# Two half-height products side by side: the low remainder of two width tiles on the two halves of TensorE's rows

## What is computed

```python
def _moe2_ref(x, domain_probs, w1, w2):          # x: 3072 x 320, E = 4, F = 1024
    p = domain_probs / (domain_probs.sum(-1, keepdims=True) + 1e-09)
    for e in range(E):
        h = np.maximum(x @ w1[e], 0.0)
        out += p[:, e:e + 1] * (h @ w2[e])
    return out
```

## Time and profile before

| | us |
|---|---|
| median of 3 runs (lowest, highest) | 1663.45 (1659.49, 1669.53) |
| profiled execution, its own time | 1664.84 |
| span of the profiled execution | 1663.1 |
| first matmul of the experts to the end of the span | 966.86 to 1663.1 |
| one steady step of the experts | 14.35 |

### The profile page before, as it was taken

The page is one execution under the profiler, slowest core; times in us unless marked ns, Lnnn a source line. Parts: engine busy times, 40 slices in busy tenths (PEclk is TensorE's granted clock), DMA queues, the critical chain, the costliest instruction groups (busy, mean ns, idle before and its releaser), DMA issues. The chain is left out here.

```text
span 1663.1 us, 37883 instructions
## 1 busy us (share of the span) xinstructions
PE 1484.1 (89%) x15888; PEld 1295.1 (78%) x15888; DVE 811.2 (49%) x1396; ACT 420.4 (25%) x859; POOL 374.4 (23%) x314
## 2 busy tenths in 40 slices
PE   2387688998989999999969779999999999999998
PEld 1266566877877877877868679999999999999998
DVE  7959765776865955853211323333333333333333
ACT  1123343343333233333223311111111111111111
POOL 4122553332332322321233340202020202020000
PEclk9978798999998988998989889999999999999999
DMA  6545684065066135111010420101010100000011
GB/s 183 163 129 144 161 216 109 17 179 145 11 161 159 31 109 133 37 56 41 9 35 1 147 70 0 35 0 35 0 35 0 34 0 18 17 0 0 0 47 47
DMA packets 89411, 112.84 MB, mean 68 GB/s; under 512 B 10952, under 2 KB 67400, under 8 KB 89288
## 3 DMA queue, kind: packets, MB, share of 16 engines
q1 hardware_dynamic: 89288, 111.05, 24.2%
HBM read 78.73 MB, written 32.28 MB: 67 GB/s over the span
## 5 line engine op out<-in xcount | busy, mean ns | idle before, releaser
L1443 PE MATMUL banks<-x2t,u 128*128 x1536 | 377.6, 393 | 8.4 <-POOL u L1410 8.4
L1453 PE MATMUL banks<-u,hid 128*128 128x320 f32 x2304 | 360.6, 309 | 0.0
L1453 PEld LDWEIGHTS banks<-u,hid 128*128 128x128 f32 x2304 | 349.0, 188 | 11.2
L1508 DVE SCALAR_TENSOR_TENSOR hid<-banks,hid 128x512 fp32r<-128x512 f32 x192 | 132.7, 691 | 414.0 <-ACT hid L1478 414.0
L1443 PEld LDWEIGHTS banks<-x2t,u 128*128 128x128 f32 x1536 | 284.2, 189 | 61.3 <-issue 8.6
L1478 ACT ACTIVATE hid<-banks 128x512 fp32r<-128x512 f32 x192 | 115.0, 599 | 581.5 <-PE banks L1443 581.5
L859 PE MATMUL banks<-xt,wi 128*128 128x512 f32 x768 | 197.6, 400 | 20.5 <-issue 12.8
L868 PE MATMUL banks<-wo,hid 128*128 128x320 f32 x1152 | 183.8, 309 | 5.6 <-POOL hid L1283 5.6
L868 PEld LDWEIGHTS banks<-wo,hid 128*128 128x128 f32 x1152 | 175.4, 188 | 14.1 <-POOL hid L1283 6.4
L859 PEld LDWEIGHTS banks<-xt,wi 128*128 128x128 f32 x768 | 142.3, 191 | 48.4 <-issue 13.9
L1283 POOL TENSOR_TENSOR hid<-shared,hid 128x512 fp32r<-128x512 f32 x96 | 123.5, 1287 | 226.8 <-ACT hid L1011 226.5
(11 more groups left out here) (112 smaller groups left out, 1553.3 us busy)
## 6 DMA issues: line engine op xcount, KB each, us to landing
scaled_operands<-made SPq DMA_DIRECT2D x41, 416.8 KB
made<-kbaw SPq DMA_DIRECT2D x41, 312.0 KB
kb<-scaled_operands SPq DMA_DIRECT2D x24, 416.0 KB
raw<-w SPq DMA_DIRECT2D x8, 640.0 KB, 5.6
lam<-scaled_operands SPq DMA_DIRECT2D x24, 209.6 KB
at<-scaled_operands SPq DMA_DIRECT2D x24, 208.0 KB
raw<-w SPq DMA_DIRECT2D x8, 512.0 KB, 4.0
rt<-rvt SPq DMA_DIRECT2D x96, 40.0 KB
```

The source lines that it names most:

```text
L1443: mm = pe.matmul(p_up[f][:], u1[:, par, w, f * 128:(f + 1) * 128], xt[:, x, cols], start=(i == 0), stop=(i == 7))
L1453: mm = pe.matmul(p_dn[t][:, 0:D], hid[:, f, h, t * 128:(t + 1) * 128], u2[:, par, w, f, :], start=(f == 0 and i == 0), stop=(f == NFU - 1 ...
L1508: dve.scalar_tensor_tensor(out=hid[:, f, 1, :], in0=p_up[f][:], scalar=0.0, in1=hid[:, f, 0, :].bitcast(F32), op0=ALU.max, op1=ALU.subtract)\
```

## The change

The pass (LO2, ST2) of every `up` is taken out, and `up` has seven passes. In its place `remainders(f)` is called once for each pair of tiles, after up 0 and after up 2: one matmul on rows 0 to 63 for tile f (low weights x `ST2`, whose upper half is the tokens' high part) and one on rows 64 to 127 for tile f + 1 (low weights x a new slot `BELOW`, whose lower half is a copy of the high part), into the two banks `p_up[f]` and `p_up[f + 1]`. The product of the low weights and the tokens' low part, which the pass before had along with it, is left out. The first of the two ends the group of tile f and signals `e_up`; the second opens the group of tile f + 1, which its `up` ends. ScalarE makes one copy more per chunk in the turning stage. TensorE's steps are written out for the six chunks and the two halves, and only the loop over the 4 experts is left.

```diff
-        xt = sb("x2t", [128, 5, NT * 128], F32R)
+        xt = sb("x2t", [128, 6, NT * 128], F32R)
...
+                    if k == 2 and c >= 2:
+                        pe.wait_ge(below_saved, c - 1)
...
-            passes = [(HI0, HI0), (HI0, LO0), (LO0, HI0), (HI1, HI1), (HI1, LO1), (LO1, HI1), (ST2, ST2), (LO2, ST2)]
+            pe.wait_ge(below_saved, NCH)
+
+            passes = [(HI0, HI0), (HI0, LO0), (LO0, HI0), (HI1, HI1), (HI1, LO1), (LO1, HI1), (ST2, ST2)]
...
-                cols = bass.ds(n * TOK, TOK)
+                cols = slice(n * TOK, (n + 1) * TOK)
...
-                                       start=(i == 0), stop=(i == 7))
-                    mm.then_inc(e_up, 1)
+                                       start=(f % 2 == 0 and i == 0), stop=(f % 2 == 1 and i == 6))
+                    if f % 2:
+                        mm.then_inc(e_up, 1)
+
+                def remainders(f):
+
+                    for s, x in ((0, ST2), (1, BELOW)):
+                        half = slice(64 * s, 64 * s + 64)
+                        mm = pe.matmul(p_up[f + s][:], u1[half, par, LO2, (f + s) * 128:(f + s + 1) * 128],
+                                       xt[half, x, cols], start=(s == 1), stop=(s == 0))
+                        if s == 0:
+                            mm.then_inc(e_up, 1)
...
                 up(0)
+                remainders(0)
                 for f in range(1, NFU):
                     up(f)
+                    if f % 2 == 0:
+                        remainders(f)
                     down(f - 1)
                 down(NFU - 1)
 
-            blocks(pe.Fori, step)
+            with pe.Fori(0, NE) as e:
+                for par in range(2):
+                    for n in range(NCH):
+                        step(e, par, n, (2 * e + par) * NCH + n)
...
+                    if k == 2:
+                        act.activation(xt[64:128, BELOW, c * TOK:(c + 1) * TOK], TURN[c % 2][k][64:128, :], ACT.Copy)\
+                            .then_inc(below_saved, 1)
```

More of the change, by code:

```diff
@@ L48 @@
 HI0, HI1, LO0, LO1, ST2, LO2 = range(6)
+BELOW = LO2
 INV_STEPS = 3 + 2 * (BLK - 1) + 1
@@ L1341, in experts @@
         cleared = sem("sum_cleared")
+        below_saved = sem("x2_remainder_below_saved")
         block = ctx.enter_context(nc.Block())
```

## The result

The changed kernel takes 1688.7 us (median of 6 runs, 1680.04 to 1692.93), the kernel before 1661.89 in the same six rounds. The ratio is 1.0156, 95% interval 1.0123 to 1.0189: slower by 1.6%, or 26.8 us. The forecast was 28.6 us on the median (1663.45 to 1692), with a range of 1669 to 1713.

A forecast was written before the change was run, and what follows sets the result against it. The prediction took TensorE to bound the experts. To the profiled 1664.84 us it added 25.9 for the pairs and 3 for the jumps, giving 1693.7, or 1692 against the median of 1663.45; range 1669 to 1713.

The forecast's parts named there:

- TensorE is the bound, and the pitch is the price: Experts: the stage ends when TensorE ends; every 0.1 us lost per pair of tiles costs 9.6 us.
- The saving, one matmul per pair: Each pair of tiles: two half-height matmuls run side by side, saving one matmul, 0.23 us.
- Way in, way out, bare load behind: Around each pair: 0.09 us in, 0.09 out, 0.11 for up 1's bare load and 0.01 for the next interval.
- The pair's own loads: Pair's two fp32r weight loads, not made ahead: 0.20 us, bounds 0 and 0.22, scaled from fp32 rows.
- The jumps: Three jumps back over twelve written-out TensorE steps: 1 us each, 3 in all, ends 0 and 6.6.
- the cover: At each far jump: TensorE's program can be past the last down early, hiding at most 2.0 us.
- the fetch: At each far jump: code fetched when asked for, up to a small transfer's landing, 2.2 us.
- The turning stage is covered: Turning stage: six more ScalarE copies add at most 3.6 us, to 963.5; PE waits until 966.86, so no cost.
- The two loads are not bare: Rival: the pair's loads are made during the way in; +0.07 us per pair, 6.7 us, 1672 with jumps; chance 0.15.
- The changes of tiling are hidden: Rival: only the pairs' saving is left, 21 us saved, 1645 after the jumps; chance 0.07.
- Not side by side in fp32r: Rival: the half-height pair doesn't overlap in fp32r; another 0.22 us per pair, 21 us, 1713; chance 0.12.
- The jumps cost more: Rival: the jumps or a late down 0 cost 10 us or more on top, 1702 and above; chance 0.07.

The follow-up runs named there:

- both on the same rows: Changed kernel with the expert loop also written out (no jumps), both half-height matmuls of a pair on rows 0 to 63: 1699.3 us against 1658.76 before.
- four at once: Changed kernel without jumps, all four half-height matmuls of a step together at its head: 1665.63 us against 1662.39 for the kernel before.
- the two kernels that have them: The changed kernel, 1688.7 us, and the kernel before with only its TensorE steps written out, expert loop kept, 1667.76 us against 1658.76.

## Why the prediction was right, and where it was off

- **TensorE is the bound, and the pitch is the price.** Right: PE had no wait in the experts but at the start and at the jumps, and the step lengths add up to the difference.
- **The saving, one matmul per pair.** Right. Both start within 0.01 us, and on the same rows it is 0.23 us more.
- **Way in, way out, bare load behind.** Right: 0.32 and 0.34 as in the earlier trace rows, where they had been read off a place with plain fp32 on the half rows. The way out, 0.43 less the load's 0.11 and the pitch of 0.23, is 0.09 as forecast, and it stands alone in two experiments (both on the same rows, four at once) with 0.32 against 0.23.
- **The pair's own loads**, the term that no row showed, was put at 0.20 and is 0.11. The step that failed is "0.11 x 0.10 / 0.06": the 0.10 us of L721 were read as two loads one behind the other, and measured against the 0.06 us of L1427 as one. With a single half-height matmul the interval is the same 0.43, so two loads on different rows are not bare for longer than one. The trace of before had it too, in the rows of the loads:

```profile
799.57 0.19 PEld L721 LDWEIGHTS banks<-rt,shared 40*128 40x128 f32 x2 [0.36 <-issue]
...
799.68 0.19 PEld L721 LDWEIGHTS banks<-rt,shared 40*128 40x128 f32 x2
...
948.25 0.14 PEld L1427 LDWEIGHTS banks<-ident,x 128*128 128x128 f32 x1
```

The first two loads of L721 start together at 799.57, and the next two 0.11 us later: its 0.10 us are one load's time, not two. What differs is L1427, a transpose, whose second load starts 0.06 us behind its first at 948.19; why that is half as long no run shows. The net loss per pair is 0.19 us instead of 0.27, 18.2 us instead of 25.9.
- **The jumps** were put at 1 us each, 3 in all, with 6.6 as the upper end, and cost 8.0 to 9.5. Both the cover and the fetch were off. The block that is fetched starts only 0.75 to 0.85 us before `up` is due, where the forecast had a cover of up to 2.0 us, and from its start to the first matmul it takes 2.6 to 3.0 us, where a small transfer had 2.2. The difference is the 1.8 to 2.2 us of wait. And a second part was not in the forecast at all: the clock. Behind three of the six jumps in the two kernels that have them TensorE ran at 0.50 for some 3 to 4 us, which cost another 1.6 or 1.7 us each. The two errors are of opposite sign (7.7 us too much, 6.5 too little). That the sum is so close, 28.6 forecast and 26.8 measured, is luck.
- **The turning stage is covered.** Right, and with 4.0 us to spare where 3.4 were forecast:

```profile
949.95 0.69 DVE L1524 TENSOR_TENSOR x2t<-banks,x2t 64x512 fp32r<-64x512 f32 x1 [0.20 <-ACT x2t L1496]
...
951.77 2.89 POOL L1412 TENSOR_TENSOR u<-raw,u 128x1280 fp32r<-128x1280 f32 x1
...
954.80 3.35 PE L1448 MATMUL banks<-x2t,u 128*128 128x512 f32 x7 [6.82 <-POOL u L1412]
```

VectorE's last subtraction ends at 950.64, POOL's split at 954.66, and PE starts at 954.80.

- **The rivals.** "The two loads are not bare" (+0.07 per pair) fell: +0.19, one load bare. (By its own terms it stood at 1663.45 + 6.7 + 3 = 1673, not 1672.) "The changes of tiling are hidden" fell: they are paid in full although the neighbours are matmuls of 512 columns. "Not side by side in fp32r" fell by the run with both on the same rows. "The jumps cost more" came true in part, with 6.5 us on top instead of 10 or more.

The Trainium skill, "TensorE: Matmul & The Clock Gate", Part 3, gives a pack the time of one matmul and some 4 ns for each further tile. The pair itself agrees (starts within 0.01 us); what it costs where it stands alone, 0.43 us to the next matmul, is more. The Trainium skill, "Runtime: NRT & Kernel Launch", Instruction fetch mechanics, has the taken branch out of what is loaded wait for a fetch. The 2 us at the far jumps and the block ahead of each agree with that.

## What to carry to other kernels

Matmuls on parts of TensorE's rows save time here only in runs: each excursion to the half rows cost 0.09 + 0.11 us on the way in and the same on the way out, 0.40 us, with one pair in it or with two. A pair of 512 columns saves 0.23. So one pair alone loses 0.17 us by these rows (0.19 by the step), and two pairs in a row, with the wait behind them moved away, gain 0.06 us. Read the way in and the way out from a place of the trace where such a change already stands, and count what follows it, not the packed matmuls alone. Look at the rows of the weight loads as well as at those of the matmuls: whose load is bare stands there. Before a loop's body is written out, ask what its jump back will have to fetch: here 12 steps cost 2 us a jump and up to 1.7 us more of low clock, 6 steps nothing.

## What the runs showed of the hardware that was not expected

- The price of a change of tiling is paid once per change, not per matmul: 0.09 us at the change and 0.11 us in the interval behind it, whatever stands there (full height behind full height 0.34 us, pair behind pair 0.34 us). A second pair in the same run paid nothing of its own.
- Loads for the two halves of the rows cost no more time than one: 0.43 us to the next matmul in both cases.
- A far jump back fetched one block of 16 KB just before its wait, and took 2.6 to 3.0 us from the start of this transfer to the first matmul, though the transfer itself lasted 0.9 to 1.4 us; a jump over six steps fetched nothing.
- TensorE is otherwise always busy in the experts. Behind three of the six far jumps, with 1.91, 2.06 and 2.06 us of idle time, its granted clock fell to 0.50 for some 3 to 4 us; behind the other three, with 1.66, 1.71 and 1.84 us, it stayed at 1.00. Six cases don't make a rule, but the loss of a short wait can be nearly twice the wait.
